# One low half of a weight behind the third difference on VectorE, in the second phase of a fused attention and experts kernel

## The reference

```python
def phi(x):                                  # attention with features, per head (4 x 8 heads, 576 rows, 64 wide)
    proj = einsum('bhsd,df->bhsf', x, w_phi) # 128 features
    proj = proj - max(abs(proj), axis=-1)
    return concatenate([exp(proj), exp(-proj)], axis=-1)
q_p, k_p = phi(q), phi(k)
kv = einsum('bhsf,bhsd->bhfd', k_p, v)
z = sum(k_p, axis=2)
x = einsum('bhsf,bhfd->bhsd', q_p, kv) / (einsum('bhsf,bhf->bhs', q_p, z) + 1e-6)
...
h = x @ w_in                                 # x: 2304 x 512, w_in: 512 x 2048
x = (h * clip(h + 3, 0, 6) / 6) @ w_out      # w_out: 2048 x 512
...
# then a gate picks one of 8 experts for each row: relu(x @ w1[e]) @ w2[e], scaled
```

## Time and profile before

| | us |
|---|---|
| median of 3 runs | 830.22 |
| lowest, highest | 828.48, 830.37 |
| profiled execution | 827.24 |
| its span | 825.6 |
| TensorE matmul busy | 802.2 (97%) |
| VectorE busy | 560.5 (68%) |
| ScalarE busy | 393.0 (48%) |
| GpSimd busy | 179.9 (22%) |

### The profile page before, as it was taken

How to read it: one execution, slowest core, us unless ns; L and a number is a source line. 1 busy time by engine, 2 the same in 40 slices (tenths; PEclk the granted TensorE clock), 3 DMA queues, 4 the chain that set the end, 5 groups by cost and what they waited for, 6 DMA issues and landing times.

```text
span 825.6 us, 19432 instructions
## 1 busy us (share of the span) xinstructions
PE 802.2 (97%) x7126; PEld 496.9 (60%) x7127; DVE 560.5 (68%) x1140; ACT 393.0 (48%) x857; POOL 179.9 (22%) x204
## 2 busy tenths in 40 slices
PE   7999999999999999999999999999999999999995
PEld 5666656655555555555555555556767777777773
DVE  5788798897978988888898897845723453222221
ACT  5888898883644644645646546434101121001110
POOL 4556666660000001010000001010211322111100
PEclk9999999999999999999999999999999999999998
DMA  7466677746656656855764756383273926266600
GB/s 237 148 204 206 213 237 207 215 143 219 233 204 217 228 206 220 262 210 207 217 253 167 246 219 208 135 343 142 83 278 142 378 65 237 78 231 248 235 28 14
DMA packets 67449, 164.37 MB, mean 199 GB/s; under 512 B 28614, under 2 KB 32966, under 8 KB 60736
## 3 DMA queue, kind: packets, MB, share of 16 engines
q1 hardware_dynamic: 61472, 146.74, 52.4%
q0 software_dynamic: 5760, 16.80, 5.7%
q10 hardware_dynamic: 160, 0.07, 0.0%
HBM read 114.16 MB, written 47.55 MB: 196 GB/s over the span
## 4 chain that ended last, share of the span: by engine, by line
PE 67%; DVE 16%; issue 10%; ACT 4%; DMA 1%; POOL 1%; SPq 1%; DVEq 0%; ACTq 0%; POOLq 0%
PE ps L909 17%; PE ps L898 15%; PE ps L994 11%; PE ps L1006 11%; PE ps L747 3%; DVE u_mx L1569 3%; DVE arena L1594 2%; PE ps L777 2%; PE ps L810 2%; DVE y_words L1561 1%; DVE arena L1320 1%; DVE arena L1337 1%; DVE relu L1650 1%; PE ps L984 1%; ACT arena L1112 1%
## 5 line engine op out<-in xcount | busy, mean ns | idle before, releaser
L898 PE MATMUL ps<-arena,w_in_sb 128*128 128x384 f16 x1152 | 200.9, 326 | 0.0
L909 PE MATMUL ps<-w_out_sb,arena 128*128 128x512 f16 x576 | 171.3, 379 | 1.5 <-DVE stage L1655 1.5
L898 PEld LDWEIGHTS ps<-arena,w_in_sb 128*128 128x128 f16 x1152 | 111.8, 98 | 81.1 <-issue 0.2
L1288 ACT ACTIVATE x_t<-ps 128x512 f16<-128x512 f32 x54 | 31.6, 596 | 200.3 <-PE ps L994 175.0
L994 PE MATMUL ps<-x_t,arena 128*128 128x128 f16 x2112 | 121.5, 219 | 2.0 <-issue 1.9
L994 PEld LDWEIGHTS ps<-x_t,arena 128*128 128x128 f16 x2112 | 119.2, 98 | 5.9 <-issue 2.6
L1006 PE MATMUL ps<-arena,x_t 128*128 128x512 f16 x528 | 117.9, 379 | 0.0
L909 PE MATMUL ps<-w_out_sb,stage 128*128 128x512 f16 x288 | 109.1, 379 | 0.0
L1260 ACT ACTIVATE arena<-relu 128x384 f16<-128x384 f32 x96 | 50.0, 521 | 119.1 <-DVE relu L1650 119.1
L909 PEld LDWEIGHTS ps<-w_out_sb,arena 128*128 128x128 f16 x576 | 55.7, 98 | 61.9 <-issue 4.8
L1762 DVE SCALAR_TENSOR_TENSOR x_t<-ps,x_t 128x512 f16<-128x512 f32 x54 | 36.7, 690 | 78.9 <-ACT x_t L1288 78.9
(11 more groups left out here) (203 smaller groups left out, 892.0 us busy)
## 6 DMA issues: line engine op xcount, KB each, us to landing
arena<-split SPq DMA_DIRECT2D x36, 1024.0 KB
arena<-in_moe_w SPq DMA_DIRECT2D x16, 2048.0 KB
split<-arena SPq DMA_DIRECT2D x16, 2048.0 KB, 7.4
arena<-in_qkt SPq DMA_DIRECT2D x15, 576.0 KB, 6.3
stage<-in_moe_w_in SPq DMA_DIRECT2D x16, 512.0 KB, 5.3
stage<-in_moe_w_out SPq DMA_DIRECT2D x16, 512.0 KB, 6.1
x_t<-rows POOLq DMA_DIRECT2D x27, 257.0 KB
y_words<-recs SPq DMA_DIRECT2D x32, 144.0 KB, 3.0
```

The source lines that it names most:

```text
L898: last = nc.tensor.matmul(ps[:, HB[f % GB], 0:BN], w_in_sb[:, lw, c, f * P:(f + 1) * P], xt[:, a, lx, c, :], start=c == 0 and lw + lx == 0 ...
L909: last = nc.tensor.matmul(ps[:, YB + r, :], g_sb[lg_][:, f % GB, r * P:(r + 1) * P], w_out_sb[:, lw, f, :], start=f == 0 and lg_ + lw == 0 ...
```

## The change

In the second phase the high half of the input weight's piece gets a function of its own, `piece_in_hi`, and stays where it was. Its low half, which stood right behind it, moves behind the third difference and `pair_out`, ahead of the low half of the output weight. The same is done in `values_pair`, where it moves behind `scales` as well. In `last_pieces` the call is added and the order stays. The first phase is not touched.

```diff
+            def piece_in_hi(u, a):
+                dve.wait_ge(stage_loaded[a], (u - a) * 16 + 32)
+                nc.vector.tensor_scalar(w_in_flat[:, 0, bass.ds((u - PAIRS // 2) * Q, Q)], stage[:, a, 0, :], s_up[:, 0:1], None,
+                                        ALU.mult).then_inc(piece_hi, 1)
+
             def piece_lo_of(u, a, w):
                 dst, cols = (w_in_flat, w_out_flat)[w], bass.ds((u - PAIRS // 2) * Q, Q)
-                if w == 0:
-                    dve.wait_ge(stage_loaded[a], (u - a) * 16 + 32)
-                    nc.vector.tensor_scalar(dst[:, 0, cols], stage[:, a, 0, :], s_up[:, 0:1], None, ALU.mult).then_inc(piece_hi, 1)
                 dve.wait_ge((piece_hi, piece_hi_out)[w], u - (PAIRS // 2 - 1))
...
             def both(u, a, phase):
-                piece = piece_lo_of if phase else piece_max_of
                 differences(u + 1, 1 - a, 1)
-                piece(u, a, 0)
+                (piece_in_hi(u, a) if phase else piece_max_of(u, a, 0))
                 differences(u + 1, 1 - a, 2)
                 pair_out(u, a)
-                piece(u, a, 1)
+                if phase:
+                    piece_lo_of(u, a, 0)
+                    piece_lo_of(u, a, 1)
+                else:
+                    piece_max_of(u, a, 1)
                 differences(u + 2, a, 0)
                 v_max(u + 2, a)
...
                 differences(u + 1, 1 - a, 1)
-                piece_lo_of(u, a, 0)
+                piece_in_hi(u, a)
                 max_over_rows(1, 1)
                 differences(u + 1, 1 - a, 2)
                 max_of(1, slice(3, 4))
                 pair_out(u, a)
                 scales(slice(3, 4))
+                piece_lo_of(u, a, 0)
                 first_x()
                 x_units()
                 piece_lo_of(u, a, 1)
...
             def last_pieces():
+                piece_in_hi(PAIRS - 1, 1)
                 for w in range(2):
                     piece_lo_of(PAIRS - 1, 1, w)
```

## The result

The changed kernel takes 831.62 us (median of 20 runs, 830.12 to 834.07), the kernel before 829.45 (20 runs, 827.47 to 832.37). The ratio is 1.0026, with a 95% interval from 1.0015 to 1.0036: slower by 2.2 us, 1.2 to 3.0. Forecast was slower by 4.2 or 4.3, at 834.5. The sign held and the time lies in the range; the size is half. Two of the signs are smaller than announced: TensorE's idle time in front of L797 is 0.54 and not 1, and against the second exponentials the third difference starts 1.20 earlier and not 1.4, since those move up by 0.25 themselves. So the question was where the other half of the loss had gone.

A forecast was written before the change was run, and what follows sets the result against it. ScalarE's and GpSimd's roads to L797 were read as nearly equal, above TensorE's floor of 10.64 us a pair. Loop +3.6 and hand-written pair +0.6 sum to +4.2, giving a median of 834.5 us, range 831.0 to 838.5.

The forecast's parts named there:

- TensorE's idle time in front of L797: Sign in the second phase's pairs: TensorE idle about 1 us a pair before L797, released by GpSimd.
- the two roads: Second-phase pairs: ScalarE's and GpSimd's chains to L797 are nearly equally long; shortening ScalarE's uncovers GpSimd's, 0.09 behind.
- (a): Second-phase pairs: third difference (L1337) starts 1.4 us earlier, at P+3.1; ScalarE can use 0.55 of it.
- The sign of 1.4: Second-phase pairs: third difference (L1337) 1.4 us earlier relative to the second exponentials' start.
- (b): Finished pair's copies move up less, waiting for TensorE's L819; L1348 at P+5.35, nobody waiting for them earlier.
- (c): Loop pairs: both low halves hit GpSimd's additions, 0.87 each; additions 5.97, loop 11.74, +3.6 over six pairs.
- The pair written out by hand: `values_pair`, pair 14: a low half now lies over additions that took 4.23; L797 moves from P+10.91 to P+11.54, +0.6.
- the last line of the sum: Adds +4.2 on a profiled execution of 827.2 us, 3.0 under the median of 830.2, giving 834.5.
- Back to back or dearer collisions: Rival, loop pairs: low halves cost 2.0 to 2.1 per pair, +6, 836.5; by the full rule 839; 12%.
- The free collision: Rival, loop pairs: input's low half costs GpSimd nothing, falling on short additions; loop 10.87, 828.5; 12%.
- The faster case: Rival, loop pairs: collisions under 0.64 a pair let the earlier third difference gain 3.2 us, 827; 6%.

The follow-up runs named there:

- search_instead: Changed kernel with VectorE waiting for L607 before first_x; in the loop a one-operand search replaces the input weight's low half: 827.85 us, ratio 1.0008.
- behind_third: Changed kernel with VectorE waiting for L607 before first_x; in the loop the input's low half stands right behind the third difference, ahead of pair_out: 831.59 us.
- pool_late: Kernel before plus one tiny GpSimd store ahead of the last pair's fourth addition, so VectorE's L1500 comes first: 829.67 us, ratio 1.0000.
- tail_before: Kernel before plus one wait: VectorE starts first_x in pair 14 only after GpSimd's L607: 826.43 us, ratio 0.9990; repeated 827.08, ratio 0.9962.
- before_again: Kernel before, unchanged, run again for noise and a second trace: 829.48 us, ratio 1.0018 to the group's other runs of it.
- after_third: Changed kernel, unedited, for a third trace: 831.46 us, ratio 1.0016 to the kernel before at 829.87.
- after_again: Changed kernel, unedited, run again: 832.12 us, ratio 1.0052 to the kernel before at 827.50.
- tail_after: Changed kernel plus one wait: VectorE starts first_x in pair 14 only after GpSimd's L607: 830.24 us, ratio 1.0032.

## Why the prediction was wrong in size and right in the rest

**What bounds the kernel now, the two roads.** Right. GpSimd's road was 0.09 behind ScalarE's, and became the bound.

**(a) and (b), the third difference and the copies.** Right in the first (P+3.08 for P+3.1). The sign of 1.4 "relative to the second exponentials" did not follow from the prediction's own sums, which move those up from P+2.37 to P+2.11; it is 1.20. The copies' L1348 came at P+5.62 instead of P+5.35, without consequence.

**(c), the price of a collision and the loop.** Right: 5.97 for 5.97, loop 11.74 for 11.74, six pairs +3.54 for +3.6. search_instead and behind_third show that the low half over the additions is the cause: a search in its place, no price; another place over the additions, the same price and 0.15 more (the prediction's "about 0.25 more" for that came without its working). Which property of the low half it is, the second operand or the large output, is not shown. Of the two roads to L797 I had left one out: TensorE's L747 now waits 0.41 for the first difference's subtraction, which stands behind the two low halves, so that the idle time in front of L797 is 0.54 and not 1 us. It costs nothing, as L607 ends later still.

**The pair written out by hand, +0.6: this step failed.** I took the one order that the earlier trace rows show, the fourth addition's turn ahead of L1500's, as the kernel's order and moved everything from there. In the three traces of the kernel before it was so in one; in the other two VectorE's turn came first. The tail then takes 18.3 or 18.5 instead of 15.4. In the changed kernel the low half stands in that place, the order is the same in all three traces, and the tail is 16.0 or 17.3. So the term is +0.6 against the cheap outcome and between −1.0 and −2.5 against the dear one. With the loop's 3.5 that is 4.1, or 1.0 to 2.5 (between the medians: 2.2, 4.6 and 1.6 in the three groups that have the changed kernel; the 4.6 is 2.6 against the other runs of that group). With the tie out of both kernels it is 3.8. The same error is in the last line of the sum, which adds the 4.2 of that one execution to a median 3.0 above it, as if the median execution had the same tail. Of the 2.9 by which 834.5 is too high, 0.8 is the median of 3 runs that it starts from (830.22, where 20 runs give 829.45). The rows to see the tie by were there: issues at 177.17 on VectorE and 177.21 on GpSimd, in a kernel of which I had just said that each excludes the other.

How often which outcome comes can't be counted, since a trace is one execution. That the groups' medians differ because of it fits all three, with pool_late equal to the kernel before in the last. What shows it is that the spread goes when the tie goes, and that the one wait alone takes 2.8 off the median in the last group; the share of it in the 2.2 of the first measurement is argued and not shown.

**The rivals.** Back to back or dearer collisions: no; GpSimd gets its turn between the two halves. (Their price should read about 2.15 by the terms given, 2.56 less 0.41, and not 2.0 to 2.1.) The free collision: no; the first low half did fall on an addition of 64 partitions, and that took 1.60 instead of 0.72. The faster case: no. The rule of the Trainium skill (SBUF — State Buffer, Who interferes with whom) is that the pair is held for the whole instruction. By that rule the loop would be 12.56, an estimate; the trace shows 11.74, so here it holds in kind and not in length.

## A version that beats both

tail_before, the kernel before with one wait: 0.9990 (0.9977 to 1.0002) and 0.9962 (0.9948 to 0.9976) of it. 826.43 and 827.08 us against 827.28 and 829.87 for the kernel before in the same groups, and 830.24 for the changed kernel even with the same wait. The first of the two intervals includes 1, so over the kernel before the gain is clear of noise in one of two measurements (5 runs with the wait); from the changed kernel its runs lie wholly apart (828.53 at most against 830.17 at least; in the other group 828.45 against 829.59 for the changed kernel with the same wait).

## What to carry to other kernels

When two engines share a resource, a move on one is paid by the other: lay the moved instruction over the other engine's timeline and count the collisions, and count them anew for what follows. The low half that seemed to delay VectorE stood where GpSimd was idle (3.31 us in front of its additions).

Where two instructions of different engines that exclude each other are issued almost together (0.04 to 0.06 us here) ahead of a critical step, one profile shows one outcome of a tie. Work out the other as a case of its own. Where one order is clearly better, force it by a wait on the engine that has time: here VectorE idled 2.82 and nothing waited for it.

A profiled execution below all timed ones (827.24 against 827.47 to 832.37) is itself a hint that it was a lucky one.

## What the runs showed of the hardware

**TensorE's clock after a short idle time is not a matter of its length alone.** After 2.40 us idle in front of L797 it fell to 0.50 in before_again and stayed at 1.00 in pool_late; after 1.84 it fell to 0.50 in after_third and stayed at 1.00 in after_again. Later in the kernel the same shows in front of one group of L994, in the changed kernel and in the kernel before, first traces (7.15 us at a clock of 0.87 to 0.92 in the stretches of 8 us around, or 5.53 at 1.00):

```profile
620.87 7.15 PE L994 MATMUL ps<-x_t,arena 128*128 128x128 f16 x96 [1.93 <-issue]
```
```profile
615.98 5.53 PE L994 MATMUL ps<-x_t,arena 128*128 128x128 f16 x96 [1.94 <-issue]
```

Idle for 1.93 and 1.94 us: once it cost 1.6 us more. In the fourteen traces this group takes 6.92 to 7.16 in six, after 1.93 to 2.55 of idle time, and 5.53 in eight, after 0.75 to 2.09. The long form is in all three traces of the changed kernel and in one of the three of the kernel before, but also in tail_before and not in tail_after. Whether the change has a hand in it, these traces can't tell. It makes the changed kernel's executions longer and not shorter, so it is not where the missing half of the loss went.

**A waiting engine gets in between two instructions of the other.** VectorE's two low halves are issued one right behind the other, and GpSimd, waiting, came in between them in the pairs of the changed kernel: the first is stretched by the addition ahead of it (1.57), the second by the one between (1.76). In the first trace the first low half ends at 123.05, the addition that waited (issued 122.05) at 123.65, the second low half (issued 122.97) at 124.73, and the last addition at 125.86. The four additions take 5.96 to 5.98 in all eighteen pairs of the loop in the three traces of the changed kernel.
